# Splitting queries and keys for a two-pass attention: GpSimd makes both low halves, a DMA copies the rounded queries

## The reference

```python
# q, k, v: (4, 8, 576, 64), s: (4, 8, 576)
scores = q @ k.transpose(0, 1, 3, 2) / sqrt(64)
cum = cumsum(maximum(s, 0), axis=-1)
scores = where(causal, -1e9, scores + minimum(-(cum[..., :, None] - cum[..., None, :]), 0))
attn = exp(scores - scores.max(-1)); attn = attn / (attn.sum(-1) + 1e-9)
x = (attn @ v) laid out as (2304 tokens, 512)
...
# then two gated layers of the MLP kind: 512 -> 1024 -> 512 and 512 -> 768 -> 512
```

## Time and profile before

| what | value |
|---|---|
| median of 3 runs | 746.23 us (745.2 to 746.96) |
| the profiled execution | 745.12 us, its span 743.3 us |
| PE busy | 709.4 us, 95% of the span |
| DVE, ACT, POOL busy | 393.9 us, 320.5 us, 253.9 us |
| DMA, queue of the kernel | 59.02 MB, 33.4% of 16 engines |
| TensorE clock granted, mean | 0.997 |

### The profile page before, as it was taken

The page is one execution under the profiler, slowest core; times in us unless marked ns, Lnnn a source line. Parts: engine busy times, 40 slices in busy tenths (PEclk is TensorE's granted clock), DMA queues, the critical chain, the costliest instruction groups (busy, mean ns, idle before and its releaser), DMA issues.

```text
span 743.3 us, 12597 instructions
## 1 busy us (share of the span) xinstructions
PE 709.4 (95%) x4248; PEld 659.3 (89%) x4248; DVE 393.9 (53%) x700; ACT 320.5 (43%) x765; POOL 253.9 (34%) x284
## 2 busy tenths in 40 slices
PE   3899999998899979999999999999999999999998
PEld 3788898887887878989898999989999999899996
DVE  6999999999868655463535446403213123032120
ACT  3888898898865334242424334212122121121211
POOL 8767678888798443524111000000000000000000
PEclk9999999999999999999999999999999999999999
DMA  8698988889664052810000031010010000100101
GB/s 182 156 210 216 193 190 190 192 189 216 147 155 98 1 130 42 206 50 1 1 1 0 1 114 57 1 43 0 1 43 1 16 27 1 42 0 0 42 0 42
DMA packets 58230, 59.47 MB, mean 80 GB/s; under 512 B 23572, under 2 KB 45204, under 8 KB 58164
## 3 DMA queue, kind: packets, MB, share of 16 engines
q1 hardware_dynamic: 58196, 59.02, 33.4%
HBM read 44.15 MB, written 10.10 MB: 73 GB/s over the span
## 4 chain that ended last, share of the span: by engine, by line
PE 71%; DVE 8%; DMA 5%; issue 5%; ACT 4%; SPq 4%; POOL 2%; DVEq 0%; ACTq 0%; POOLq 0%
PE ps L675 10%; PE ps L674 10%; PE ps L673 10%; PE ps L593 4%; PE ps L592 4%; PE ps L591 4%; PE ps L518 3%; PE ps L520 3%; PE ps L519 3%; PE ps L689 3%; PE ps L690 3%; PE ps L688 3%; DMA qk_raw<-in_qk_dram 3%; PE ps L484 3%; DVE nmax L1085 2%
## 5 line engine op out<-in xcount | busy, mean ns | idle before, releaser
L675 PE MATMUL ps<-x_lo,w_hi 128*128 (+1 forms) x432 | 144.4, 334 | 0.0
L673 PE MATMUL ps<-x_hi,w_hi 128*128 128x384 f32 x432 | 144.3, 334 | 0.0
L674 PE MATMUL ps<-x_hi,w_lo 128*128 128x384 f32 x432 | 144.3, 334 | 0.0
L873 ACT ACTIVATE probs<-ps,nmax 128x576 f32<-128x576 f32 (+4 forms) x160 | 82.7, 536 | 6.7 <-DVE nmax L1085 6.7
L484 PE MATMUL ps<-ident,probs 128*128 128x128 f32 x480 | 75.7, 282 | 9.9 <-DVE pt_lo L1092 7.2
L1092 DVE TENSOR_TENSOR pt_lo<-ps,pt_hi 128x512 fp32r<-128x512 f32 (+1 forms) x128 | 78.2, 652 | 6.8 <-ACT pt_hi L883 3.1
L674 PEld LDWEIGHTS ps<-x_hi,w_lo 128*128 128x128 f32 x432 | 81.1, 188 | 0.2
L673 PEld LDWEIGHTS ps<-x_hi,w_hi 128*128 128x128 f32 x432 | 81.1, 188 | 0.2
L675 PEld LDWEIGHTS ps<-x_lo,w_hi 128*128 128x128 f32 x432 | 81.1, 188 | 0.0
L466 PE MATMUL ps<-k_a,q_a 128*128 128x288 f32 (+2 forms) x192 | 63.1, 336 | 14.4 <-DMA qk_b<-setup 10.8
L883 ACT ACTIVATE pt_hi<-ps 128x512 fp32r<-128x512 f32 (+1 forms) x128 | 69.7, 573 | 12.8 <-PE ps L484 10.6
(11 more groups left out here) (100 smaller groups left out, 1424.8 us busy)
## 6 DMA issues: line engine op xcount, KB each, us to landing
qk_raw<-in_qk_dram SPq DMA_DIRECT2D x64, 288.0 KB, 4.4
xT<-halves SPq DMA_DIRECT2D x32, 144.0 KB, 2.4
xb_dram<-halves SPq DMA_DIRECT2D x32, 144.0 KB, 2.5
xb<-xb_dram SPq DMA_DIRECT2D x24, 192.0 KB, 3.6
rinvB<-rsum_dram SPq DMA_DIRECT2D x24, 192.0 KB, 4.5
stage<-in_moe_w_dram SPq DMA_DIRECT2D x18, 256.0 KB, 4.6
out_dram<-stage SPq DMA_DIRECT2D x18, 256.0 KB, 2.0
v_raw<-in_v_dram SPq DMA_DIRECT2D x32, 128.0 KB, 4.0
```

The source lines that it names most:

```text
L673: pe.matmul(dst, w_hi[f][:, i, c, :], x2_hi[par][:, c, :], start=(c == 0), stop=False)
L674: pe.matmul(dst, w_lo[f][:, i, c, :], x2_hi[par][:, c, :], start=False, stop=False)
L675: mm = pe.matmul(dst, w_hi[f][:, i, c, :], x2_lo[:, c, bass.ds(g * GT, GT)], start=False, stop=(c == KC - 1))
L873: act.activation(dst, SCORES[c], ACT.Exp, bias=nmax[par][:, c:c + 1], accum_out=sums_all[:, c, bass.ds(t, 1)]).then_inc(exp_done, 1)
```

## The change

The host lays the 64 rows of queries and keys down twice in DRAM, so that one transfer fills all 128 rows of `qk_raw`. GpSimd multiplies by a column of per-row factors in place of a constant: `q_a` rows 0 to 63 are the rounded scaled queries, rows 64 to 127 at first the rounded unscaled queries; for `k_a` it is the other way round (the scale is 1/8, so that the product is the same). GpSimd then subtracts in rows 64 to 127 to get the low half of the queries, and makes the low half of the keys as before. It no longer writes `q_b`: SP issues a transfer from rows 0 to 63 of `q_a` into those of `q_b` (`copy_q`). DVE fills the two columns of factors at the start and does nothing more for queries.

```diff
-                for copy in range(2):
-                    dst = qk_raw[par][D * copy:D * (copy + 1), :, :].rearrange("p i s -> p (i s)")
-                    sp.dma_start(dst, rows).then_inc(qk_loaded[par], 16)
+                sp.dma_start(qk_raw[par][:, :, :].rearrange("p i s -> p (i s)"), rows).then_inc(qk_loaded[par], 16)
+            def copy_q(h, par):
+                sp.wait_ge(q_hi_ready, h + 1)
+                sp.dma_start(f32(q_b[par][0:D, PAD:SP]), f32(q_a[par][0:D, PAD:SP])).then_inc(aux_loaded[par], 16)
...
             sp.wait_ge(rows_zeroed, 2)
+            copy_q(0, 0)
             sp.wait_ge(cum_ready, 2)
...
             def reload(t, par, known=None):
+                if known != 2:
+                    copy_q(t - 2, par)
                 sp.wait_ge(k_hi_ready, t - 1)
...
             reload(HEADS - 1, 1)
+            copy_q(HEADS - 2, 0)
             sp.wait_ge(rinv_done, 1)
             store_rinv(slice(0, LAST))
             reload_aux(HEADS - 1, 1)
             reload_v(HEADS - 2, 0)
             sp.wait_ge(rinv_stored, 16 * NCH)
+            copy_q(HEADS - 1, 1)
             load_rinv(0)
...
-                pe.wait_ge(aux_loaded[par], (t - par) * 8 + 16)
+                pe.wait_ge(aux_loaded[par], (t - par) * 16 + 32)
...
-                pool.tensor_scalar(q_a[par][:, PAD:SP], q_raw[par][:, :], SCALE, 1.0, ALU.mult, ALU.mult).then_inc(q_hi_ready, 1)
-                pool.tensor_scalar(k_a[par][:, :], k_raw[par][:, :], 1.0, 1.0, ALU.mult, ALU.mult).then_inc(k_hi_ready, 1)
-                pool.tensor_scalar(q_b[par][0:D, PAD:SP], q_raw[par][0:D, :], SCALE, 1.0, ALU.mult, ALU.mult)
-            def k_low(t, par):
+                pool.tensor_scalar(q_a[par][:, PAD:SP], q_raw[par][:, :], q_scale[:, :], 1.0, ALU.mult, ALU.mult).then_inc(q_hi_ready, 1)
+                pool.tensor_scalar(k_a[par][:, :], k_raw[par][:, :], k_scale[:, :], 1.0, ALU.mult, ALU.mult).then_inc(k_hi_ready, 1)
+            def qk_low(t, par):
+                pool.wait_ge(q_hi_ready, t + 1)
                 pool.wait_ge(k_hi_ready, t + 1)
+                pool.tensor_tensor(q_a[par][D:P, PAD:SP], q_raw[par][D:P, :], f32(q_a[par][D:P, PAD:SP]), ALU.subtract).then_inc(q_lo_ready, 1)
+                pool.wait_ge(q_lo_ready, t + 1)
                 pool.tensor_tensor(k_b[par][0:D, :], k_raw[par][0:D, :], f32(k_a[par][0:D, :]), ALU.subtract).then_inc(k_lo_ready, 1)
...
-            def q_low(t, par):
-                dve.wait_ge(q_hi_ready, t + 1)
-                dve.scalar_tensor_tensor(out=q_a[par][D:P, PAD:SP], in0=q_raw[par][D:P, :], scalar=SCALE,
-                                         in1=f32(q_a[par][D:P, PAD:SP]), op0=ALU.mult,
-                                         op1=ALU.subtract).then_inc(q_lo_ready, 1)
...
+    laid["qk"] = _np.concatenate([laid["qk"], laid["qk"]], axis=1)
```

More of the change, by code:

```diff
@@ L38, in attention_and_mlp @@
     HEADS, D, _, S = qkT.shape
+    D //= 2
     DM, FF = w_in.shape
@@ L103, in attention_and_mlp @@
         one = sb(keep, "one", [P, 1])
+        q_scale = sb(keep, "q_scale", [P, 1])
+        k_scale = sb(keep, "k_scale", [P, 1])
         x_ = ExitStack()
@@ L182, in attention_and_mlp @@
         rows_zeroed = sem("rows_zeroed")
+        scales_set = sem("scales_set")
         setup_dve = sem("setup_dve")
@@ L734, in qk_high @@
             def qk_high(t, par, known):
-                pool.wait_ge(qk_loaded[par], (t - par) * 16 + 32)
+                pool.wait_ge(qk_loaded[par], (t - par) * 8 + 16)
                 if known is None or known >= 2:
@@ L753, in _ @@
             pool.wait_ge(rows_zeroed, 2)
+            pool.wait_ge(scales_set, 2)
             pool.sem_inc(pool_passed, 1)
             qk_high(0, 0, 0)
-            k_low(0, 0)
+            qk_low(0, 0)
             pool.wait_ge(setup_pool, 7)
@@ L769, in slot @@
                     qk_high(t + 1, 1 - par, None if known is None else known + 1)
-                    k_low(t + 1, 1 - par)
+                    qk_low(t + 1, 1 - par)
                 if live(known, 1):
@@ L1056, in _ @@
         def _(dve):
+            for lo, hi, scale in ((SCALE, 1.0, q_scale), (1.0, SCALE, k_scale)):
+                dve.memset(scale[0:D, :], lo)
+                dve.memset(scale[D:P, :], hi).then_inc(scales_set, 1)
             for row in one_rows:
@@ L1101, in invert_sums @@
                 dve.reciprocal(flat, flat).then_inc(rinv_done, 1)
-            q_low(0, 0)
             for i in range(2):
@@ L1118, in slot @@
             def slot(t, par, known):
-                if live(known, -1):
-                    q_low(t + 1, 1 - par)
                 if live(known, 0):
```

## The result

| | before | changed |
|---|---|---|
| median | 745.72 us (744.72 to 746.96, 4 runs) | 810.28 us (807.25 to 811.95, 4 runs) |
| profiled execution: span, mean granted clock | 743.3 us, 0.997 | 810.1 us, 0.960 |

The ratio is 1.0851, with a 95% interval of 1.0833 to 1.0870: slower by 64.6 us. The forecast was 789, range 776 to 815.

What follows compares the result with a forecast made beforehand. The prediction saw TensorE and DVE nearly full before, and the late copy of queries binding after: + 41.8 us over heads 4 to 30, + 43.2 with the other parts, on 745.12, plus 1.1 to the median: 789 us, range 776 to 815.

Steps and rivals of the forecast that it cites:

- It comes too late in every slot: SP's list: the copy is issued 0.6 or 1.1 us before scores_4 needs it, but takes 2.4 us to land.
- The sum: Heads 4 to 30, bound by the copy loop: 212.2 us against 170.4, + 41.8; with the other parts + 43.2.
- rivals 3 and 4: 3: copy lands late behind stores and weight piece, 820 to 841, chance 0.07; 4: TensorE's clock falls, 808 or 847, chance 0.07.
- `scores_4` to store: Loop's first two steps: scores_4 start to ScalarE's copy, 2.14 us, then to SP's first store, 1.07 us.
- rival 4: TensorE's clock falls in waits for the copy: + 58, 847, in every head; + 19, 808, in a third; chance 0.07.
- the one that likened the coming waits to that of 182 to 185 us: TensorE's coming waits, except head 27's, are like the one there, where the clock stayed at 1.00.
- landing: Loop's last step: the copy lands 2.4 us after issue, TensorE starts 0.1 later; + 2.6 in all for four 512 KB pieces.
- store to issue: SP's list, first store to the copy's issue: 1.5 us without a weight piece, 2.5 with one.
- the next bound: GpSimd during weight splitting: 6.5 to 7.0 us per head, hidden under the copy's mean of 7.7, otherwise binding.
- Rival 1: At scores_4 the copy is in time and DVE's relief counts: up to 11.1 us faster, down to 735; chance 0.03.
- Rival 2: The copy is in time and GpSimd binds: 8 pairs of heads at 13 to 14 us, about 750; chance 0.03.
- One load in place of two: counted at nothing.: Raw-data load: same bytes, one issue fewer, which the copy takes back; hidden behind the copy loop, no gain or loss.

Runs made afterwards that it cites:

- 1: The changed kernel with the copy of the rounded queries two stores further up in SP's list: 755.7 us, ratio 1.011.
- 4: The kernel before with only the copy from q_a to q_b, at the change's place in SP's list, instead of GpSimd's third multiplication: 810.9 us.
- experiment 3: The changed kernel plus 8 or 24 matmuls that nobody reads, right ahead of scores_4 in TensorE's list: 796.3 us.
- 10: The changed kernel with aux load and copy ahead of the values in SP's list, and the xb loads behind the last head's reload: 752.6 us, ratio 1.005.
- 7: The kernel before with one raw-data transfer of 128 rows per head in place of two of 64, nothing else: 742.95 us, ratio 0.9944.

## Why the prediction was right, point by point

- **The place and the mechanism.** "It comes too late in every slot", and the loop from `scores_4` over the store to the copy: shown by the times of heads 4 to 28, by 1 (moving the copy removes it) and by 4 (the copy alone makes it).
- **The sum.** Forecast + 41.8 us for heads 4 to 30; measured 234.0 us for these intervals against 170.4, + 63.6. Forecast at the start + 0.8, measured + 1.4 (head 3 at 29.57 against 28.14); at the end + 0.6, measured + 1.8. The sum was short by 21 us of 65. The forecast's own range, 780 to 806, was missed; the stated one held, near its upper end, because it had been widened for milder forms of rivals 3 and 4, and both came true in part. The terms:
  - *`scores_4` to store*, 2.14 + 1.07: near it in 16 intervals (2.82 to 3.24) and short by 1.1 to 1.6 us in 11, where the clock had fallen: 15.5 us (experiment 3 takes 14.7 off this step). The prediction had this as rival 4, at a chance of 0.07, with 19 us "in a third" of the heads. The failed step is the one that likened the coming waits to that of 182 to 185 us: those were 1.4 us, but behind a weight piece they are 2.55 to 5.8, most of them 2.7 to 2.9, by the prediction's own terms an interval of 8.2 in which TensorE has some 5.8 us of work, so that 2.4 us of waiting already followed from its sum, where its text said 0.9 to 2. The waits in rounds without a piece, 0.2 to 1.4 us, left the clock up; those behind a piece brought it down in 10 of 12 cases (not before heads 9 and 21, whose waits were 3.10 and 2.81).
  - *landing*, taken as 2.4 and 0.1: 2.63 in slots without a weight piece, 3.02 on average behind a piece of 256 KB, 3.5 to 6.1 behind one of 512 KB. About 12 us short. The prediction added about 0.6 for each of the four large pieces; they wanted 1.0 to 3.6, and it added nothing for the small ones, which wanted 0.5.
  - *store to issue*, taken as 1.5 and 2.5: measured 1.30 and 2.31 on average, some 4.5 us too much. That this took off a part of what the other two lacked is luck.
- **GpSimd.** Forecast 6.5 to 7.0 us per head with splitting and "the next bound": 13.13 us per pair from head 18 on in 1 and 10, 6.57 per head. The column of factors cost 0.74 against 0.67 us, and each wait for the predecessor 0.16.
- **Rival 1**, the copy in time and a gain by DVE: it did not happen, and 1 shows that even an early copy gives no gain with this division of work. Its price, up to 11 us faster, left out that GpSimd takes the relief away. **Rival 2**, about 750 with GpSimd as the bound, is near what 1 and 10 gave, 755.7 and 752.6, but GpSimd bound only their second half; in 1 more of the loss was the copy landing late.
- **"One load in place of two: counted at nothing."** Under the loop nothing speaks against it (810.9 without it and without the moved work, 810.3 with both; no run separates the two). In the kernel before it is worth some 4 us by the ratio of 7, 2.8 between the profiled executions. The step that calls it hidden fits this kernel and would have been wrong for the load alone: without the loop its 0.9 us at the start and its 1.8 us over 27 heads reach the end.

## What to carry to other kernels

A transfer that replaces a cheap instruction inherits its place in a queue: ask first what the issuing queue waits for ahead of it, and whether that wait hangs on the previous round of the consumer, since then a latency becomes a loop. Price the wait that such a loop makes also for TensorE's clock, per kind of round and not on average: a wait twice as long in every other round cost more than its own length. When a change has several parts, time them alone; here the loser carried a part that wins.

## What the runs showed of the hardware

- In the changed kernel waits of TensorE of 0.2 to 1.4 us left the granted clock at 1.00. Waits of 2.55 to 5.8 us behind a weight piece brought it to 0.50 in 10 of 12 rounds (one of 3.10 and one of 2.81 did not), and one of 5.08 behind the loads of xb did too. In experiments 1 and 3 it also came down once each, behind a wait of 2.05 and one of 1.87, so that the length of a wait alone doesn't decide it in these runs. In the changed kernel it was back at 1.00 before the next `scores_4`, in a stretch of busy TensorE. Filling a part of the wait with unread matmuls kept it at 1.00 (experiment 3, 140 to 160 us) and made the kernel 14 us faster. The Trainium skill, "TensorE: Matmul & The Clock Gate", section "HAM oscillation — how this bites in real kernels", describes this form of loss, a clock that falls again in each round's wait for a DMA; this case agrees in 10 of 12 rounds.
- With one transfer over 128 partitions for queries and keys the DMA engines were busy 71.6% of 20 to 200 us, where two of 64 made it 84.6%, at nearly the same bytes (34.79 and 34.33 MB). The Trainium skill, "SBUF — State Buffer", section "Can I just issue two DMAs to hit both halves?", says that only one transfer over all 128 partitions can use all the ports; the busy shares fit that, though no run here shows the ports.
- DVE's low half of the queries (L1078, two inputs in SBUF) took 0.755 to 2.034 us in the kernel before, median 1.172. GpSimd's subtractions of 64 rows took 1.388 to 1.430 us in the changed kernel, without that instruction beside them; the one of the kernel before took up to 1.940, but in the kernel of 7, where DVE's instruction runs as well, at most 1.451. The Trainium skill, "SBUF — State Buffer", section "Who interferes with whom", says that a DVE instruction with two SBUF inputs contends with a GpSimd instruction that reads SBUF. DVE's spread fits that; no run here shows that it is the cause.
- An issue on SP, 0.3 to 0.6 us as a rule, took 1.71 and 2.63 us in the changed kernel for the raw load that followed the first and the second weight piece of 512 KB and the copy (row: ns min/median/max):

```profile
L292 SPq DMA_DIRECT2D qk_raw<-in_qk_dram x32: 333/375/2633, 1.2 to 255.4; - x32
```

Why the first two of four such issues were long and the later ones not, no run here settles.
